# Bias stage of an attention and gated-FFN kernel: one of four feature sets on GpSimd, every third bias copy on VectorE

## The reference

```python
psi_rel = np.log1p(np.abs(rel))                       # rel = query position - key position
psi_i = np.log1p(np.maximum(pos[:, None], 1.0))
x = (psi_rel / psi_i)[..., None]
h = np.maximum(x @ w1 + b1, 0.0)                      # 32 hidden features for each pair of positions
bias = h @ w2                                         # 8 heads
scores = scores + bias.transpose(2, 0, 1)[None, :, :, :]
```

## Time and profile before

| what | value |
|---|---|
| median of 3 runs | 774.19 us |
| profiled execution: its time, its span | 776.97 us, 775.1 us |
| PE busy | 742.2 us (96%) |
| DVE busy | 516.8 us (67%) |
| ACT busy | 458.5 us (59%) |
| POOL busy | 353.4 us (46%) |

### The profile page before, as it was taken

How to read it: one execution, slowest core, us unless ns; L and a number is a source line. 1 busy time by engine, 2 the same in 40 slices (tenths; PEclk the granted TensorE clock), 3 DMA queues, 4 the chain that set the end, 5 groups by cost and what they waited for, 6 DMA issues and landing times. The chain is left out here.

```text
span 775.1 us, 14693 instructions
## 1 busy us (share of the span) xinstructions
PE 742.2 (96%) x5092; PEld 606.7 (78%) x5092; DVE 516.8 (67%) x1084; ACT 458.5 (59%) x938; POOL 353.4 (46%) x481
## 2 busy tenths in 40 slices
PE   7788999999999999998979999999999999999998
PEld 4336777777777767678868998899899889989996
DVE  6996777777777777655980687687158677814851
ACT  6996776776677677657621765275257436625730
POOL 0002554455467787964581461656045255503600
PEclk9998999999999999999999999999999999999999
DMA  6898133232263321116110114122011412200102
GB/s 157 182 222 179 44 79 79 66 75 70 62 197 78 85 64 48 38 43 227 55 54 1 55 61 157 67 71 82 1 56 54 163 55 64 74 28 27 55 1 82
DMA packets 92888, 63.15 MB, mean 81 GB/s; under 512 B 60432, under 2 KB 86160, under 8 KB 92816
## 3 DMA queue, kind: packets, MB, share of 16 engines
q1 hardware_dynamic: 92384, 62.13, 29.3%
q10 hardware_dynamic: 432, 0.09, 0.1%
HBM read 42.15 MB, written 9.44 MB: 67 GB/s over the span
## 5 line engine op out<-in xcount | busy, mean ns | idle before, releaser
L1331 PE MATMUL z_ps<-xc,wc 128*128 128x384 f32 x864 | 165.5, 336 | 2.7 <-ACT keep L778 2.6
L580 POOL TENSOR_SCALAR probs<-probs,recip 128x512 f32<-128x512 f32 x128 | 88.6, 692 | 154.9 <-DVE recip L976 154.9
L1331 PEld LDWEIGHTS z_ps<-xc,wc 128*128 128x128 f32 x864 | 150.5, 188 | 6.6 <-issue 2.8
L751 ACT ACTIVATE probs<-neg_scores,neg_max 128x576 f32<-128x576 f32 x144 | 111.1, 772 | 61.5 <-DVE neg_max L956 61.5
L606 POOL TENSOR_TENSOR wc<-t_raw,wc 128x512 fp32r<-128x512 f32 x37 | 48.6, 1314 | 109.8 <-ACT wc L770 109.8
L956 DVE CUSTOM_DVE_ANT_0 neg_scores<-so_ps,bias 128x576 f32<-128x576 f32 x128 | 91.9, 756 | 3.9 <-PE so_ps L1212 3.2
L1395 PE MATMUL f_ps<-wo_h,h_h 128*128 128x512 f32 x216 | 85.8, 397 | 5.3 <-DVE h_l L1048 3.0
L1331 PE MATMUL y_ps<-xc,wc 128*128 128x384 f32 x432 | 86.8, 335 | 3.3 <-DVE sig L1032 3.1
L1395 PE MATMUL f_ps<-wo_h,h_l 128*128 128x512 f32 x216 | 85.3, 395 | 0.0
L1395 PE MATMUL f_ps<-wo_l,h_h 128*128 128x512 f32 x216 | 85.3, 395 | 0.0
L778 ACT ACTIVATE keep<-z_ps 128x384 f32<-128x384 f32 x108 | 52.9, 490 | 54.6 <-PE z_ps L1331 53.8
(11 more groups left out here) (120 smaller groups left out, 1503.2 us busy)
## 6 DMA issues: line engine op xcount, KB each, us to landing
w_stage<-in_w_gate SPq DMA_DIRECT2D x18, 512.0 KB, 3.5
w_stage<-in_w_val SPq DMA_DIRECT2D x18, 512.0 KB, 3.5
bias<-bias_rows SPq DMA_DIRECT2D x12, 576.0 KB, 7.0
out<-out_sb SPq DMA_DIRECT2D x18, 256.0 KB, 2.0
q_raw<-in_q SPq DMA_DIRECT2D x32, 128.0 KB, 2.7
k_raw<-in_k SPq DMA_DIRECT2D x32, 128.0 KB, 2.6
v_main<-in_v SPq DMA_DIRECT2D x32, 128.0 KB, 2.4
x_whole<-attn_transposed SPq DMA_DIRECT2D x9, 384.0 KB, 5.2
```

Source lines behind the costliest of these rows:

```text
L580: nc.gpsimd.tensor_scalar(row[:, 0:NT * P], row[:, 0:NT * P], by, 1.0, ALU.mult, ALU.mult).then_inc(normed, 1)
L751: nc.scalar.activation(probs[s % RING][:, place, :], neg_scores[:, place, :], ACT.Exp, bias=neg_max[:, stat(s, place)], scale=-1.0, accum_ ...
L1331: last = nc.tensor.matmul(quad_ps[bank][n % 2][:, 0:CH], wc[:, n % 2, wl, W_PARTS.index(wp), t, :], xc[:, X_PARTS.index(x), xl, t, :], sta ...
```

## The change

`POOL_SET = SETS - 2`: set 2 of each unit is made by GpSimd, and VectorE makes sets 0 and 1. Of the units 2, 5, 8, ... 35 VectorE makes the copy out of PSUM (12 of 36); ScalarE keeps the others. `bias_copied` becomes `act_copied` and `dve_copied`, and those who waited for the former (the next user of the PSUM banks, the stores on the SP queue, the start of the attention) wait for the one or the other, or for both. In VectorE's list the copy of unit `u - 1` stands behind the features of unit `u`.

```diff
+        def dve_copies(units):
+            return units // 3
...
             def store_bias(d):
                 i = d % ROW_BUFS
-                sp.wait_ge(bias_copied, 2 * d + 2)
+                sp.wait_ge(act_copied, 2 * d + 2 - dve_copies(2 * d + 2))
+                if dve_copies(2 * d + 2):
+                    sp.wait_ge(dve_copied, dve_copies(2 * d + 2))
...
+            pool.wait_ge(slopes_ready, 2)
+            pool.wait_ge(log_win_in, 16)
+            for u in range(UNITS):
+                if u >= 2:
+                    pool.wait_ge(bias_summed, u - 1)
+                if u == MAIN_UNITS // 2:
+                    pool.wait_ge(tail_win_in, 16)
+                col = u * SETS + POOL_SET
+                nc.gpsimd.tensor_scalar(feats[u % 2][:, POOL_SET, :], window(u, POOL_SET), slopes[:, col:col + 1],
+                                        neg_b1[:, 0:1], ALU.mult, ALU.max).then_inc(feats_pool, 1)
...
                 if u + 1 < UNITS:
                     relu_feats(u + 1)
-                copy_bias(u)
+                if dve_copies(u + 1) == dve_copies(u):
+                    copy_bias(u)
...
-                for j in range(RELU_SET):
+                for j in range(POOL_SET):
...
+            def copy_bias(u):
+                d = u // 2
+                dve.wait_ge(const_ready, 2)
+                dve.wait_ge(bias_summed, u + 1)
+                if d >= ROW_BUFS:
+                    dve.wait_ge(bias_stored[d % ROW_BUFS], duo_stored(d - ROW_BUFS))
+                nc.vector.tensor_scalar(bias_rows[d % ROW_BUFS][:, u % 2, :].rearrange("p (a n) -> p a n", a=2),
+                                        bias_ps(u % 2), float(D ** 0.5), head_const[:, 0:1],
+                                        ALU.mult, ALU.add).then_inc(dve_copied, 1)
...
                 max_feats(u)
+                if u and dve_copies(u) > dve_copies(u - 1):
+                    copy_bias(u - 1)
+            if dve_copies(UNITS) > dve_copies(UNITS - 1):
+                copy_bias(UNITS - 1)
...
             def bias_unit(u):
                 if u >= 2:
-                    pe.wait_ge(bias_copied, u - 1)
-                pe.wait_ge(feats_ready, (u + 1) * RELU_SET)
+                    if dve_copies(u - 1) > dve_copies(u - 2):
+                        pe.wait_ge(dve_copied, dve_copies(u - 1))
+                    else:
+                        pe.wait_ge(act_copied, u - 1 - dve_copies(u - 1))
+                pe.wait_ge(feats_ready, (u + 1) * POOL_SET)
+                pe.wait_ge(feats_pool, u + 1)
                 pe.wait_ge(feats_relu, u + 1)
```

More of the change, by code:

```diff
@@ L144, in program @@
         feats_relu = sem("feats_relu")
+        feats_pool = sem("feats_pool")
         bias_summed = sem("bias_summed")
-        bias_copied = sem("bias_copied")
+        act_copied = sem("act_copied")
+        dve_copied = sem("dve_copied")
         bias_stored = [sem(f"bias_stored{i}") for i in range(ROW_BUFS)]
@@ L294, in program @@
         RELU_SET = SETS - 1
+        POOL_SET = SETS - 2
         RELU_ROWS = RELU_SET * GRP * H
@@ L715, in copy_bias @@
                 act.wait_ge(bias_summed, u + 1)
-                if d >= ROW_BUFS and u % 2 == 0:
+                if d >= ROW_BUFS:
                     act.wait_ge(bias_stored[d % ROW_BUFS], duo_stored(d - ROW_BUFS))
@@ L719, in copy_bias @@
                                      bias_ps(u % 2), ACT.Identity, bias=head_const[:, 0:1],
-                                     scale=float(D ** 0.5)).then_inc(bias_copied, 1)
+                                     scale=float(D ** 0.5)).then_inc(act_copied, 1)
             def high_q(pair):
@@ L1346, in _ @@
                 bias_unit(u)
-            pe.wait_ge(bias_copied, UNITS)
+            pe.wait_ge(act_copied, UNITS - dve_copies(UNITS))
+            pe.wait_ge(dve_copied, dve_copies(UNITS))
             for s in range(STEPS + DRAIN):
```

## The result

The changed kernel has a median of 816.39 us over 6 runs (814.41 to 818.68), the kernel before 774.57 us over its 6 (770.41 to 777.61). The ratio is 1.0535, with an interval of 1.0507 to 1.0563. I had forecast 777.0 us and a range up to 784. The prediction was wrong, and by far more than any of its rivals allowed: the worst of them stood at 783.9 us.

The account below looks back on a forecast made before the run. VectorE was taken to bound the bias stage: 3.64 us of own work plus two 0.50 us collisions per three units, 1.547 against 1.470 us a unit, 36 units, +2.8 us on 774.2, so 777.0 us; range 770 to 784.

Parts of the forecast that it names:

- VectorE sets the pace now, ScalarE is close behind: Bias stage before the change: VectorE's three features take 1.48 us of a 1.47 us unit, ScalarE's work 1.39 us.
- The cost of GpSimd's instruction: Bias stage: GpSimd's new 576-element, two-operand feature instruction takes about 0.82 us, its 36 costing the attention nothing.
- The order of the waits: Bias stage: copies and features waiting in turn on TensorE hold the pace at 1.44 us a unit or slower.
- The ring of 1.44 us a unit: Bias stage: wait chains of 2.78, 2.78 and 3.07 us close over six units in 8.63 us; alone worth 1.2 us.
- Collisions: Bias stage: VectorE's features and GpSimd take turns at SBUF, two collisions per three units, 0.50 us each (0.42 to 0.61).
- A microsecond in the stage is one at the end: Bias stage: TensorE is always busy from 76 us, so time gained or lost in the stage reaches the kernel's end.
- The turn lasts for the whole instruction: Rival, bias stage: each collision costs VectorE GpSimd's full 0.79 us; 1.74 us a unit, +9.7 us, 783.9 us; chance 0.06.
- The clock: Rival: TensorE's low clock at 69 to 76 us may go (-3.4 us) or enter the bias stage (2.4 us units); chance 0.06.

Follow-up runs that it names:

- e2: Kernel before plus only the copies' part: VectorE makes all three sets and every third copy, GpSimd none; 785.17 us, ratio 1.0087 to the kernel before.
- p1_probe: Kernel before with GpSimd instructions added behind the last store, alone and beside VectorE's features; alone, multiply/multiply with two operands took 0.817 us, multiply/max 2.28 us.
- e4: Changed kernel with GpSimd's set by multiply/multiply (other values) and all copies back on ScalarE; 777.68 us against 776.99 for the kernel before, ratio 1.0010.
- e5: Changed kernel, but GpSimd makes set 2 of every third unit only, into four own buffers, ScalarE all copies; 780.79 us against 776.99 before, ratio 1.0056.
- e1: Changed kernel with GpSimd's multiply/max replaced by multiply/multiply (other values for that set); 777.81 us against 777.44 for the kernel before, ratio 1.0017.
- p2_probe: Kernel before with more GpSimd operation pairs behind the last store, alone and beside VectorE's copies and splits; multiply/subtract and add/add took 2.29 us.

## Why the prediction was wrong, step by step

- *VectorE sets the pace now, ScalarE is close behind.* Borne out: adding the copies alone to VectorE gave 1.72 us a unit where its own work says 1.73 (e2).
- *The cost of GpSimd's instruction.* This is the step that failed: "GpSimd's 576 elements with two operands take about 0.745 + 0.07 = 0.82 us". The rows it came from the earlier trace rows are multiply/multiply. The estimate is right for that pair (0.817 us in p1_probe) and wrong by 2.8 times for multiply/max (2.28 alone, 2.47 in the kernel). I matched engine, instruction name and size, and did not look at the two operations in the source line. From this price followed the wrong bound: VectorE and the order of waits instead of GpSimd. With 2.55 us a unit for GpSimd (91.8/36) the sum is 36 x (2.55 - 1.47) = 38.9 us; 37.6 were measured in the stage.
- *No rival had GpSimd as the bound.* All prices for its instruction came from one family of rows, so no term went beyond 0.82 us for it. The nearest other row, a two-tile GpSimd instruction of 512 elements with 1.3 us, would have moved that end only to 1.5 us; the honest remark was that no row shows this operation at all.
- *The order of the waits.* The ring of 1.44 us a unit was not tested by itself. e4 ran at 1.44 with VectorE full, which neither proves nor refutes it. e5's last units (1.45 us each, VectorE waiting 0.36 us in three units) show that waits can hold the pace there; the one they show, VectorE waiting until TensorE releases a feature buffer, I had not listed.
- *Collisions.* Borne out once GpSimd is fast (e1): two for three units, the copy covers the third, 0.43 us each where I took 0.50 within 0.42 to 0.61. 4.54 us for three units were measured, 4.64 forecast; ratio 1.0017 measured, 1.0036 forecast. In the change itself this term decided nothing. The copy took 0.82 us where I had put 0.75, and 0.72 from start to start where I had put 0.68: a small miss.
- *A microsecond in the stage is one at the end.* Borne out for the large effects: 37.6 us in the stage of 41.8, and for e2 8.0 us there against 7.7 between the medians. e4's 2.1 us did not reach the end.
- *The turn lasts for the whole instruction.* The Trainium skill's rule (SBUF — State Buffer, "SBUF: two separate sides") says that the one who comes first blocks the other for the whole instruction. Here GpSimd's multiply/max lasts 2.70 us beside VectorE's features, and none of those took longer than 1.08 us in the probe: two of four run at full speed in its midst. The fast pair takes 0.43 to 0.50 us from VectorE, also less than its 0.82. The measurement decides: the sharing is real, but it is not by whole instructions.
- *GpSimd's speed.* The Trainium skill (GPSIMD Engine Reference, "4.1 Engine selection") calls one-input elementwise work on GpSimd roughly line rate, and names max beside add and multiply. The traces agree for multiply/multiply and disagree for multiply/max: 576 elements in 0.745 us and 512 in 0.692 are 0.83 ns for an element more, while multiply/max needs 3.3 ns.
- *The clock.* What this rival named did happen: low stretches came into the stage, and a unit took 2.15 us in them. They decided nothing, since GpSimd had only 0.8 us of slack. Its price for the stretch at 69 us, 3.4 us, was too high. p2_probe has the same instructions as the kernel before up to the last store, and its profiled execution had the full clock (1.00) from 62 to 90 us. From the first score to the last value copy it took 283.6 us against 285.3, so the low stretch cost 1.7 us. It also comes and goes from one execution to another.

So the change could not have won here. With the pair of operations that it needs, GpSimd is the bound at 2.55 us a unit. Used so little that it is not (e5), each of its instructions takes 0.76 to 0.79 us from VectorE and saves 0.49. Even the fast pair (e1, e4) only breaks even, 0.43 to 0.45 us taken for 0.49 saved. No run here beat the kernel before.

## What to carry to other kernels

A duration from a trace is that of its operation, not only of its engine, instruction name and size: before pricing a new instruction by an old row, read both source lines and compare the operations; if no row has them, say that the price is unknown, put that engine among the possible bounds, and measure the instruction by itself first. Work given to GpSimd beside VectorE's SBUF-to-SBUF work is not free for VectorE: count what a collision takes against what the moved instruction saved (0.43 to 0.83 us against 0.49 here). Where one engine is the bound, what another loses is hidden behind it (0.9%, 5.1% and 5.4% for the copies, GpSimd's set and both), so test the parts singly before blaming one.

## What the runs showed of the hardware

- GpSimd's one-input TENSOR_SCALAR on fp32, 128x576, alone: multiply/multiply 0.817 us, multiply/add 0.817, but multiply/max, multiply/min, max/multiply, multiply/subtract and add/add 2.28 to 2.29, and one operation alone (multiply or max) 1.72. A multiply by itself is slower than a multiply with a second one behind it.
- VectorE's one-input SBUF-to-SBUF feature instruction is stretched beside GpSimd (0.57 us alone, up to 1.08 in p1_probe), while its copies out of PSUM are not (0.741 to 0.750 us in p2_probe, GpSimd at 0.819).
- In p1_probe a long GpSimd instruction (multiply/max, 2.70 us) stretches only the features at its start and end; those in its midst keep 0.57 us. It takes 0.83 us from VectorE in all, and a short one (multiply/multiply) takes 0.50 in the same probe.
- Beside VectorE's instructions with two SBUF inputs GpSimd's multiply/multiply went from 0.82 to 2.20 us, the largest stretch in this study, while 14 of VectorE's 20 stayed at 0.68 and six took 1.15.
- The low stretch of the clock at the start of the attention comes and goes between executions of the same instructions: clock 0.51 from 69 to 76 us and 285.3 us from the first score to the last value copy in the kernel before, clock 1.00 and 283.6 us in p2_probe.
